# Attention's opening from unstacked parts: the first pair's rows in two products, the first stacks by transfers, keys and memory a pair later

## What is computed

```python
# q, k, v: (4, 8, 576, 64); M_prev: (4, 8, 64, 64); z_prev: (4, 8, 64); beta: (8)
scores = scale * np.matmul(q, k.transpose(0, 1, 3, 2))      # causal, softmax over keys
local = np.matmul(a, v)
q_p = phi(q)                                                # where(x > 0, x, exp(x) - 1) + 1
mem_out = einsum('bhsd,bhde->bhse', q_p, M_prev) / (einsum('bhsd,bhd->bhs', q_p, z_prev)[..., None] + 1e-06)
attn = g * mem_out + (1 - g) * local                        # g = sigmoid(beta) of the head
x = moe(attn)    # 2304 tokens, 512 -> 2048 -> 512, s * relu(h)**2 + b
out = moe2(x)    # 512 -> 1024 -> 512, softmax gate and layer norm
```

## Time and profile before

| | us |
|---|---|
| median of three runs | 821.49 |
| the profiled execution | 821.17 |
| its span, from first to last instruction | 819.4 |
| TensorE busy | 810.7 (99%) |
| VectorE busy | 510.4 (62%) |
| ScalarE busy | 339.6 (41%) |
| GpSimd busy | 339.1 (41%) |

### The profile page before, as it was taken

One profiled execution on the slowest core, in us unless ns is written; L12 is line 12 of the kernel. 1 busy time (PEld: TensorE's weight loads), 2 busy tenths in 40 slices (PEclk: granted clock), 3 DMA queues, 4 the chain that ended last, 5 costly groups with the idle time before them and its releaser, 6 DMA issues.

```text
span 819.4 us, 14574 instructions
## 1 busy us (share of the span) xinstructions
PE 810.7 (99%) x5630; PEld 704.2 (86%) x5630; DVE 510.4 (62%) x1052; ACT 339.6 (41%) x608; POOL 339.1 (41%) x453
## 2 busy tenths in 40 slices
PE   8999999999999999999999999999999999999998
PEld 7788888888888888888888899999998888888886
DVE  7877777776588653333433353346688977777762
ACT  6766776675422232222322232233436434333431
POOL 6667676676899930000000000005268844443300
PEclk9999999999999999999999999999999999999999
DMA  8587777866134320000000000000111000000001
GB/s 152 128 178 154 173 167 155 178 142 144 53 103 116 95 73 1 1 1 0 1 1 0 1 1 1 1 1 1 52 51 52 26 27 26 26 14 27 26 14 51
DMA packets 86371, 49.45 MB, mean 60 GB/s; under 512 B 65056, under 2 KB 73248, under 8 KB 86304
## 3 DMA queue, kind: packets, MB, share of 16 engines
q1 hardware_dynamic: 83760, 47.94, 24.3%
q10 hardware_dynamic: 2544, 0.59, 0.4%
HBM read 27.28 MB, written 4.72 MB: 39 GB/s over the span
## 4 chain that ended last, share of the span: by engine, by line
PE 96%; DVE 1%; issue 0%; ACT 0%; POOL 0%; POOLq 0%
PE ps_h L1297 8%; PE ps_y L1313 8%; PE ps_h L1298 8%; PE ps_h L1299 8%; PE ps_y L1314 8%; PE ps_y L1312 8%; PE ps_v L678 5%; PE ps_s L591 4%; PE ps_r L1766 4%; PE ps_r L1764 4%; PE ps_r L1765 4%; PE ps_hid L1701 4%; PE ps_hid L1699 4%; PE ps_hid L1700 3%; PE ps_x L657 3%; PE ps_x L658 3%
## 5 line engine op out<-in xcount | busy, mean ns | idle before, releaser
L1414 DVE TENSOR_TENSOR xT<-xT 128x512 f32<-128x512 f32 (+1 forms) x80 | 61.2, 765 | 127.7 <-ACT xT L1372 127.7
L1598 POOL TENSOR_TENSOR win<-stage,win 128x512 fp32r<-128x512 f32 x2 | 2.6, 1296 | 282.4 <-ACT win L1833 282.4
L1314 PE MATMUL ps_y<-g_hi,wout 128*128 128x512 f32 (+1 forms) x320 | 117.5, 367 | 0.0
L1313 PE MATMUL ps_y<-g_lo,wout 128*128 128x512 f32 (+1 forms) x320 | 117.5, 367 | 0.0
L1312 PE MATMUL ps_y<-g_hi,wout 128*128 128x512 f32 (+1 forms) x320 | 117.4, 367 | 0.0
L1378 ACT ACTIVATE g_hi<-xT 128x512 fp32r<-128x512 f32 (+1 forms) x80 | 47.3, 591 | 135.0 <-DVE xT L1416 135.0
L1297 PE MATMUL ps_h<-x_hi,win 128*128 128x512 f32 (+1 forms) x280 | 103.0, 368 | 0.0
L1299 PE MATMUL ps_h<-x_hi,win 128*128 128x512 f32 (+1 forms) x280 | 102.8, 367 | 0.0
L1298 PE MATMUL ps_h<-x_lo,win 128*128 128x512 f32 (+1 forms) x280 | 102.8, 367 | 0.0
L1372 ACT ACTIVATE xT<-ps_h 128x512 f32<-128x512 f32 (+1 forms) x80 | 44.3, 554 | 139.0 <-PE ps_h L1299 137.2
L1419 DVE TENSOR_TENSOR g_lo<-xT,g_hi 128x512 fp32r<-128x512 f32 (+1 forms) x80 | 65.1, 813 | 52.6 <-ACT g_hi L1378 52.6
(11 more groups left out here) (220 smaller groups left out, 1814.6 us busy)
## 6 DMA issues: line engine op xcount, KB each, us to landing
stacked<-cut SPq DMA_DIRECT2D x56, 288.0 KB, 4.8
out<-res SPq DMA_DIRECT2D x18, 256.0 KB, 2.0
v_raw<-in_v SPq DMA_DIRECT2D x32, 128.0 KB, 2.7
stage<-in_moe_w_in SPq DMA_DIRECT2D x16, 256.0 KB, 2.8
stage<-in_moe_w_out SPq DMA_DIRECT2D x16, 256.0 KB, 2.7
k_raw<-in_k SPq DMA_DIRECT2D x28, 128.0 KB, 2.6
q_raw<-in_q SPq DMA_DIRECT2D x28, 128.0 KB, 3.6
stage<-in_moe_w_in SPq DMA_DIRECT2D x4, 512.0 KB, 3.5
```

The costliest lines, as they stand in the source:

```text
L1313: pe.matmul(out, wout[:, f, HI, w], g_lo[:, r, 0:n], start=False, stop=False)
L1314: ins = pe.matmul(out, wout[:, f, LO, w], g_hi[:, r, 0:n], start=False, stop=(f == FT - 1))
L1414: dve.tensor_tensor(r, r, r, ALU.mult).then_inc(square_done, 1)
```

## The change

What it does, by engine:

- **Loads of pairs 0 and 1.** Raw tiles have two columns again. Keys and queries of pair 0 are issued half by SP, half by ScalarE; those of pair 1 by SP, queries first. Values of pair 0 come directly behind (one head of them from ScalarE).
- **No crossed turns.** `turn_swapped`, `double`, `put`, `low_queries` and what waits on them are gone. Pair 0 goes through `cut[0]` like later pairs: ScalarE rounds keys and queries (`round_keys(0)`, `round_first_queries`), VectorE takes the low queries (`first_low_queries`), GpSimd does it for pair 1.
- **Rows of heads 0 and 1** are made by `rows_in_two` from `cut[0]`: over 64 partitions, high queries by high keys and low queries by high keys, two products where there was one.
- **Stacks 0 and 1** are made by `stack`, four transfers each, on SP's queue. The crossings of heads 0 and 1, and the rows of heads 2 and 3, wait for them.
- **Loads of pair 2 and the memory** stand behind these on SP's queue, and so does all that follows.
- **Keys and memory a pair later.** `steps` starts at head 6; keys are turned two pairs ahead, not three, the memory is that of the own pair. Waits at `turn_output` and `memory` are moved accordingly. `feature_relu` moves between exponentials 0 and 1 of an odd head. `spent` and `cut` are placed before `mask`, so that ScalarE's start of the next layer waits for the last low keys and stacks and no more for the last memory.
- **On ScalarE the gates come first**, on VectorE too.
- The warm-up has six products, the group between three.

The diff, cut to its core:

```diff
-    DIRECT = 2
+    RAW = 2
-    WARM, WARM_BETWEEN = 10, 5
+    WARM, WARM_BETWEEN = 6, 3
...
         def stack(p):
-            sp.wait_ge(k_hi_done, p - DIRECT + 1)
-            sp.wait_ge(q_lo_done, p - DIRECT + 1)
+            sp.wait_ge(k_hi_done, p + 1)
+            sp.wait_ge(q_lo_done, p + 1)
...
-        load_keys(0)
+        head_tiles(sp, first_k[0], k, 0, 0, k_in[0])
+        head_tiles(sp, first_q[0], q, 0, 0, q_in[0])
+        last_tiles(sp, first_q[0], q, 0, q_in[0])
+        load_queries(1)
         load_keys(1)
+        sp.wait_ge(cleared, FOR_VALUES)
+        sp.wait_ge(cleared_dve, DVE_CLEARS)
+        head_tiles(sp, v_raw[0], v, 0, 1, v_in[0])
+        last_tiles(sp, v_raw[0], v, 0, v_in[0])
+        sp.wait_ge(qT_turned, 1)
+        head_tiles(sp, q_raw[0], q, 2, 0, q_in[0])
+        stack(0)
+        head_tiles(sp, q_raw[0], q, 2, 1, q_in[0])
+        last_tiles(sp, q_raw[0], q, 2, q_in[0])
+        stack(1)
         load_keys(2)
-        load_queries(2)
         load_memory()
-        load_values(0)
+        load_queries(3)
+        stack(2)
         load_keys(3)
-        load_queries(3)
         load_values(1)
-        stack(2)
         load_keys(4)
...
+        def rows_in_two(h, t, part):
+
+            mine, n = MINE[h], keys[t]
+            for lo, hi in ((0, min(n, 512)), (512, n)):
+                if lo < hi:
+                    ins = pe.matmul(ps_s[0:rows_of[t], S_AT[t] + lo:S_AT[t] + hi],
+                                    cut[0][mine, part, P * t:P * t + rows_of[t]], cut[0][mine, K_HI, lo:hi],
+                                    start=(part == Q_HI), stop=(part == Q_LO), skip_group_check=True,
+                                    tile_position=(mine.start, 0))
+            return ins
...
         def turn_output(p):
             pe.wait_ge(x_done, p + 1)
             pe.wait_ge(qT_copied, min(p + 5, NPAIR))
-            pe.wait_ge(t_mem_done, min(p + 3, NPAIR))
-            pe.wait_ge(k_lo_done, min(p + 6, NPAIR))
+            pe.wait_ge(t_mem_done, min(p + 2, NPAIR))
+            pe.wait_ge(k_lo_done, min(p + 5, NPAIR))
...
         def memory(p):
             pe.wait_ge(phi_done, p + 1)
             pe.wait_ge(m_in, 16 * 4)
-            pe.wait_ge(k_lo_done, min(p + 3, NPAIR))
+            pe.wait_ge(k_lo_done, max(4, min(p + 3, NPAIR)))
...
             if c == 0:
                 pe.wait_ge(neg_spread, h + 1)
+                pe.wait_ge(q_again, p + 1)
+                if p == 0:
+                    pe.wait_ge(stack_landed[0][h], 16 * STACK_DMAS)
...
-        act_placed(pe, 0, "k_moved0")
-        dve_placed(pe, 0, "k_moved1")
         keep_warm(ps_x[:, 0, 0:P])
-        first_rows(0)
+        first_rows_in_two(0)
+        turn_queries(1)
+        other_rows_in_two(0)
         turn_keys(1)
-        turn_queries(1)
-        third_rows(0)
-        turn_swapped_queries(1)
+        first_rows_in_two(1)
...
+        open_gates()
+        round_keys(0)
+        round_first_queries()
+        copy_queries(0)
...
                 if here:
                     exp_weights(h, 0)
+                    if not even and is_pair(pr + 1):
+                        feature_relu(pr + 1)
                     exp_weights(h, 1)
...
-                if not even and is_pair(pr + 1) and pr + 1 > 0:
-                    memory(pr + 1)
+                if not even and is_pair(pr):
+                    memory(pr)
```

619 lines of the change are left out of this document (292 added, 327 removed).

## The result

The changed kernel takes 833.54 us (median of 4 runs, 832.43 to 834.8), the kernel before on the same chip 821.4 (821.2 to 821.53). The ratio is 1.0148 (95% interval 1.0131 to 1.0166): **12.1 us slower**, where 7.0 were forecast and the range ended at 831.8. The profiled execution took 833.49 us with a span of 831.6, against 819.4: 12.2 us, and all but 0.3 of them arise in its first 232 us.

A forecast was written before the change was run, and what follows sets the result against it. TensorE, full from 60.3 us on, and before that SP's queue feeding it, were taken as the bound; 0.45 + 3.5 + 1.7 + 0.95 + 0.4 = 7.0 us slower than 821.49 gave 828.4, range 823.8 to 831.8.

The forecast's parts named there:

- Up to head 3: Opening to head 3's crossing: 2.05 us gained early are lost waiting for keys 3, and 0.45 more.
- part 2: SP's longer line of transfers: stack 2 begins at 29.4, keys 3 land at 39.9, TensorE waits 4 us.
- part 1: Up to the first crossing: first maximum at 10.05, first crossing at 15.9 instead of 17.95, 2.05 us earlier.
- rival C: TensorE's clock falls in idle stretches of the opening; one at half clock costs 2.25 us: 830.6; chance 0.12.
- Owed work: At head 3's crossing, memory of two pairs and rows of heads 4 and 5 still to do: 3.5 us.
- That keys and memory run a pair later costs nothing by itself: Whole loop: keys and memory a pair later add no time; the last ones are paid at the end.
- Waits up to the loop: From head 3 to the loop: waits for low keys 3 and stack 3, net 1.7 us more.
- the 1.0 for stack 3: Before the loop: stack 3's even head lands at 51 to 51.5, asked for at 50.5, 1.0 us of waiting.
- The loop: Rectifications between exponentials 0 and 1 delay the crossing in heads 27 and 29, 0.2 us twice: 0.4.
- With a turn of queries ahead it is hidden: Odd heads with a turn of queries (0.64 us) ahead: the moved rectifications cost nothing.
- The end: End of attention: output turn of pair 14 waits for VectorE's scaling of the last memory, 0.95 us TensorE idle.
- Rule against row: SP's queue: the skill's rule of small issue time against measured slow issues behind a stack; the forecast followed the row.

The follow-up runs named there:

- e5_lastmem: Changed kernel with the last pair's memory product moved ahead of the values of head 30: 833.27 us.
- e1_warm: Changed kernel with the earlier kernel's warm-up, 10 matmuls ahead of the first turn and 5 between instead of 6 and 3: 834.28 us.
- e3_keys: Changed kernel with SP sending keys 3 ahead of queries 3 and the third stack instead of behind both: 832.88 us.
- e6_fill: Changed kernel with 6 warm-up matmuls ahead of head 0's first crossing and 11 ahead of the wait for keys 3: 833.65 us.
- e7_spare: Changed kernel with warm-up 10 and 5 and spare matmuls in every wait of the opening, 12 of them ahead of keys 3: 834.76 us.
- e2c_relu: Changed kernel with the two rectifications of each odd head from 7 on done one head earlier on ScalarE: 832.46 us.
- e10_act: Changed kernel with the second, third and fourth stacks issued from ScalarE's queue and the rest of SP's list closed up: 835.20 us.
- e12_order: Changed kernel with SP's list reordered: keys 3 ahead of queries 3 and third stack, fourth stack ahead of keys 4, values 2, keys 5: 833.09 us.
- e13_both: Changed kernel with e12_order's SP order and e7_spare's spare matmuls, 4 instead of 12 ahead of keys 3: 831.24 us.
- e16_best: Changed kernel with e12_order, e2c_relu, gates behind the first maxima, warm-up 8 and 5, spare matmuls ahead of heads 0 and 2 alone: 828.30 us.
- e17_nospare: e16_best with the change's own warm-up of 6 and 3 and no spare matmuls: 830.05 us.
- e9_nomem: Changed kernel without the transfers of M_prev and z_prev, so the memory tiles stay zero: 833.56 us.

## Why the prediction was wrong

The direction and the main mechanisms held; the sum fell short by 5.1 us. Term by term:

- **Up to head 3: +0.45 forecast, +2.60 found.** This is the first failed step, and it failed in part 2, at stack 2: sent at 31.43, forecast 29.4. What follows it was right (keys 3 landed 10.7 us later, forecast 10.5). Of the 2.0 us, 0.75 are the late first stack (10.50, forecast 9.75): part 1 put no time for the gates on VectorE, where they took 1.9 us ahead of the low parts. 0.7 are SP's own line (20.35 us to the end of queries 3, forecast 19.65). 0.6 are the wait for keys 2 and low queries 2, made late by TensorE at half clock; I had SP's line alone decide. The clock itself, kept as rival C at 0.12 and for one idle stretch, was at 1.2 GHz for 20 us more than in the kernel before; up to head 3 it cost at most that 0.6, since TensorE still waited 2.7 us for keys 3 (forecast 4). At the upper level and with early gates (e5_lastmem) head 0 was at 15.56, forecast 15.9; part 1 behind the first maximum was sized right (5.85 us forecast, 6.0 found in e1_warm and e5_lastmem, 7.35 with the change). Head 3 at 40.77 in e5_lastmem against my 40.5 is in part luck: its first stack went 0.7 us earlier than I had it, and TensorE was at half clock from 15.5 to 29.2 us.
- **Owed work: 3.5.** It fits at its three places, but only as a difference: no run takes it out, and the turn of keys cost 0.83 us in its step, not 0.64. That keys and memory run a pair later costs nothing by itself was right as far as TensorE's own work goes.
- **Waits up to the loop: +1.7 forecast, 2.6 found** (4.32 less 1.7 owed there), of another make. TensorE's idle time in this stretch grew by 0.6 us only (1.35 instead of 0.72): memory 0 waited 1.09 us for low keys 3 (2.0 in e3_keys and e6_fill, at the upper level, the value I had), and the 1.0 for stack 3 did not come, though it did in e7_spare and e6_fill (1.2 and 1.5). The rest is mostly the 3.4 us at 1.2 GHz, some 1.7 us as an estimate from half the clock.
- **The loop: +0.4 forecast, +2.04 found.** "With a turn of queries ahead it is hidden" was the failed step. I looked at exponential 1 and at the crossing behind it, and not at the copy of queries queued behind both rectifications, nor at who waits for that copy: the memory product, which overwrites the bank. That is 0.17 us in each of the ten odd heads from 7 to 25, 1.7 in all; the 0.4 that I had for heads 27 and 29 came (0.27 and 0.12). e2c_relu gave all of it back.
- **The end: +0.95 forecast, 1.07 found** as idle time ahead of output 14's turn. The size is right; moving the product away won only 0.15 (e5_lastmem), so it is no price that can be had back by itself.
- **Rule against row.** SP was not ahead of its transfers: from the first stack at 10.5 us to the fourth at 48.7 its queue had one gap over 0.15 us with the change (0.6, ahead of the third stack), with issues of 1.4 to 2.8 us behind every stack. The row was right. The Trainium skill (DMA: Bandwidth & Descriptors, "Issuing engines are not separate DMA queues") says that the time to initiate a DMA is "usually small relative to the DMA itself"; an issue of a stack took 0.6 to 1.55 us here and its landing 3.4 to 6.0, so it was not small for a queue with this much under way. In e10_act a second queue did not help: the median landing of its stacks was 6.5 us instead of 5.1.

What the opening's loss is made of is not settled. By the medians, clock alone (e7_spare) gives nothing, order alone (e12_order) 0.4 us, both 2.3 (e13_both; the intervals, 1.0108 to 1.0141 against 1.0131 to 1.0166, still touch). With the rectifications and the gates it is 5.2 (e16_best, intervals apart), of which 2.0 are the loop's. But e17_nospare, with nothing for the clock, is already 3.5 below the change, and order, gates and rectifications one by one sum to 3.2. So the times fit a plain sum with something for the clock on top as well as they fit an interaction; for the interaction speak the traces: stack 2 left at 30.68 with the clock kept (e7_spare, SP's own line) and at 32.34 with that line shortened (e9_nomem, GpSimd's low queries 2), against 31.43. What is left in e16_best's profiled execution, 5.6 us at the next part's first matmul (225.86 against 220.22), is owed work and end, 3.5 and 1.2 by the sum above, and 0.9 more. Which work in the new opening loses the clock is open: it fell behind waits (e1_warm), but it also fell at 12.6 us behind 3.4 us in which TensorE was busy for 2.79 with nothing longer than 0.3 us between, among them products over half the partitions. A version with full-height products in the same order was not tried.
